# Moving part of an attention prologue from VectorE to GpSimd, the next scores a place later, and constant matmuls in front of the first products

## The reference

```python
q_d, k_d, v_d = mean over groups of 4 positions
out_up = repeat(softmax(scale * q_d @ k_d.T) @ v_d, 4)          # "down" part
scores = where(abs(i - j) < 4, scale * q @ k.T, -1e9)           # "local" part
x = out_up + softmax(scores) @ v                                # 2304 tokens x 512
x = (silu(x @ w_gate) * (x @ w_val)) @ w_out                    # 512 -> 1536 -> 512
h = x @ w_in
out = (maximum(h, 0) + alpha * minimum(h, 0)) @ w_out2          # 512 -> 2048 -> 512
```

## Time and profile before

| | |
|---|---|
| time, median of 3 runs | 984.84 us (984.21 to 985.62) |
| profiled execution | 983.52 us |
| its span, first to last instruction | 981.7 us |
| instructions | 20376 |
| TensorE busy | 952.8 us |
| VectorE busy | 549.7 us |
| ScalarE busy | 247.0 us |
| GpSimd busy | 134.1 us |

### The profile page before, as it was taken

The page is one execution under the profiler, slowest core; times in us unless marked ns, Lnnn a source line. Parts: engine busy times, 40 slices in busy tenths (PEclk is TensorE's granted clock), DMA queues, the critical chain, the costliest instruction groups (busy, mean ns, idle before and its releaser), DMA issues.

```text
span 981.7 us, 20376 instructions
## 1 busy us (share of the span) xinstructions
PE 952.8 (97%) x7912; PEld 889.7 (91%) x7912; DVE 549.7 (56%) x1171; ACT 247.0 (25%) x631; POOL 134.1 (14%) x151
## 2 busy tenths in 40 slices
PE   5899999899998999999999999999999999999998
PEld 3799999799997999999999999999999999999997
DVE  8777666566665666666564554444444444444443
ACT  3444222222221322222223541111111111111111
POOL 5576010010100101000013850000000000000000
PEclk9999999999999999999999999999999999999999
DMA  8465221221211211312105530010010100100000
GB/s 257 138 189 160 81 70 49 66 68 48 85 57 41 92 49 40 102 58 76 48 13 174 163 119 2 1 65 1 0 64 0 43 21 0 64 0 0 32 0 33
DMA packets 31735, 63.07 MB, mean 64 GB/s; under 512 B 2992, under 2 KB 14256, under 8 KB 31664
## 3 DMA queue, kind: packets, MB, share of 16 engines
q1 hardware_dynamic: 31664, 62.02, 20.0%
HBM read 52.57 MB, written 9.44 MB: 63 GB/s over the span
## 4 chain that ended last, share of the span: by engine, by line
PE 90%; DVE 3%; DMA 2%; issue 2%; POOL 2%; ACT 1%; SPq 0%; DVEq 0%; ACTq 0%; POOLq 0%
PE ps L975 50%; PE ps L1012 20%; PE ps L995 14%; PE ps L930 2%; DMA w_raw<-w 2%; PE ps L878 1%; POOL w_lo L428 1%; PE ps L886 1%; PE ps L938 1%; PE ps L916 1%; DMA qk<-qk 0%; DVE h_lo L806 0%; DVE qk_d_early L646 0%; DVE turned_alone L712 0%; DVE turned_one L712 0%
## 5 line engine op out<-in xcount | busy, mean ns | idle before, releaser
L975 PE MATMUL ps<-x_hi,w_hi 128*128 128x288 f32 x768 | 234.3, 305 | 0.7 <-DVE gated L816 0.2
L975 PE MATMUL ps<-x_lo,w_hi 128*128 128x288 f32 x768 | 228.7, 298 | 0.0
L975 PE MATMUL ps<-x_hi,w_lo 128*128 128x288 f32 x768 | 227.6, 296 | 0.0
L552 ACT CAST h_hi<-hidden 128x288 fp32r<-128x288 f32 (+1 forms) x192 | 90.9, 473 | 405.6 <-DVE hidden L843 332.0
L806 DVE TENSOR_TENSOR h_lo<-hidden,h_hi 128x288 fp32r<-128x288 f32 (+1 forms) x192 | 112.2, 585 | 70.0 <-ACT h_hi L552 66.8
L975 PEld LDWEIGHTS ps<-x_hi,w_hi 128*128 128x128 f32 x768 | 146.0, 190 | 4.8 <-issue 1.1
L841 DVE TENSOR_SCALAR gated<-ps,alpha_sb 128x384 f32<-128x384 f32 x96 | 59.3, 617 | 159.5 <-PE ps L975 159.5
L975 PEld LDWEIGHTS ps<-x_hi,w_lo 128*128 128x128 f32 x768 | 146.4, 191 | 0.0
L975 PEld LDWEIGHTS ps<-x_lo,w_hi 128*128 128x128 f32 x768 | 146.4, 191 | 0.0
L995 PE MATMUL ps<-h_hi,w_hi 128*128 128x288 f32 x384 | 115.6, 301 | 0.1
L1012 PE MATMUL ps<-w_lo,h_hi 128*128 128x512 f32 x288 | 113.2, 393 | 0.0
(11 more groups left out here) (123 smaller groups left out, 1423.1 us busy)
## 6 DMA issues: line engine op xcount, KB each, us to landing
w_raw<-w SPq DMA_DIRECT2D x68, 256.0 KB, 2.7
qk<-qk SPq DMA_DIRECT2D x30, 436.0 KB, 3.5
vsrc_one<-vsrc SPq DMA_DIRECT2D x29, 288.0 KB
vwin<-vwin SPq DMA_DIRECT2D x30, 192.0 KB, 2.3
y_t<-y_sb SPq DMA_DIRECT2D x8, 576.0 KB, 3.4
x_raw<-y_t SPq DMA_DIRECT2D x6, 768.0 KB, 5.6
out<-y_sb SPq DMA_DIRECT2D x5, 768.0 KB, 4.1
qk_early<-qk SPq DMA_DIRECT2D x2, 436.0 KB, 6.1
```

The lines of the kernel that those rows point to most:

```text
L552: nc.scalar.copy(h_hi[r][:, 0:width], hidden[r][:, 0:width]).then_inc(h_hi_ready, 1)
L975: mm = nc.tensor.matmul(out_ps, w[:, piece, 128 * k:128 * k + 128], x_parts[low][:, k, :], start=(k == 0 and n == 0), stop=(k == KC - 1 an ...
```

## The change

- **GpSimd averages v** of pairs 2 and 3 of the prologue (`POOL_AVERAGES`), each in two additions: halves of the groups of four in place (512 elements a partition), then the two results (256 elements). They stand ahead of `normalise(2)` and behind `normalise(3)` in its queue.
- **GpSimd makes the low parts of x** of pairs 0, 1 and 2, between the low parts of the weight pieces. TensorE waits for them with a semaphore of their own (`x_lo_early`) ahead of the loop.
- **VectorE's order** in the prologue: `turn_local` of pairs 1, 2 and 3 and the fourth `reciprocals` come forward, `average_v` of pairs 0 and 1 stands behind; `average_qk` for the next block comes behind the last low part of x. `add_up` waits for the one before it.
- **The scores of pair 0 of every next block** come at place 1 instead of 0, behind the first gate products; its maxima, exponentials and reciprocals also go a place later. `average_v`, `turn_local`, `transpose_down` and `pair_outputs` keep their places.
- **Constant matmuls**: 8 ahead of the outputs of pair 3 in the prologue, 12 behind them, into a PSUM bank that is free.

```diff
+WARM_LAST_PAIR, WARM_FIRST_GATE = 8, 12
+POOL_AVERAGES = 2
+def scored_at(k):
+    return 0 if k else 1
...
 GpSimd, prologue:
-            for k in range(PAIRS):
-                normalise(k, k, 0)
-            for j in range(POOL_PIECES, EARLY_PIECES):
-                split_rest(j)
+            def average_v(k):
+                pool.wait_ge(vsrc_in[k], 16)
+                v = vsrc_sb[0][k]
+                nc.gpsimd.tensor_tensor(v[:, :, :, 0:2], v[:, :, :, 0:2], v[:, :, :, 2:4], ALU.add).then_inc(v_halved, 1)
+                pool.wait_ge(v_halved, k - POOL_AVERAGES + 1)
+                nc.gpsimd.tensor_tensor(v_d[0][k][:, :, :], v[:, :, :, 0], v[:, :, :, 1], ALU.add).then_inc(v_averaged_pool, 1)
+            def split_x_lo(k):
+                pool.wait_ge(x_hi_ready, k + 1)
+                nc.gpsimd.tensor_tensor(x_lo[0][:, k, :], x_f32[0][k][:, :], x_hi[0][:, k, :].bitcast(F32), ALU.subtract).then_inc(x_lo_early, 1)
+            normalise(0, 0, 0)
+            normalise(1, 1, 0)
+            average_v(2)
+            normalise(2, 2, 0)
+            normalise(3, 3, 0)
+            average_v(3)
+            split_rest(2)
+            for k in range(PAIRS - 1):
+                split_x_lo(k)
+                split_rest(3 + k)
...
 ScalarE, VectorE, TensorE, attention(a, half, p):
-                if at == 1:
+                if at == scored_at(k) + 1:
...
-                if at == 0:
+                if at == scored_at(k):
...
-                if at == 2:
+                if at == scored_at(k) + 2:
...
 VectorE, add_up:
+                if not mode and k:
+                    dve.wait_ge(x_added, k)
...
 VectorE, prologue:
             reciprocals(0, 2, 0)
-            average_v(0, 0)
             turn_local(0, 1, 0)
             reciprocals(0, 3, 0)
+            average_v(0, 0)
+            turn_local(0, 2, 0)
             average_v(0, 1)
             add_up(0, 0, 0)
-            turn_local(0, 2, 0)
-            average_v(0, 2)
-            split_x_lo(0, 0, 0, 0)
+            turn_local(0, 3, 0)
             add_up(0, 1, 0)
-            turn_local(0, 3, 0)
-            average_v(0, 3)
-            split_x_lo(1, 0, 1, 0)
             add_up(0, 2, 0)
-            average_qk(1, 0)
-            split_x_lo(2, 0, 2, 0)
             add_up(0, 3, 0)
             split_x_lo(3, 0, 3, 0)
+            average_qk(1, 0)
+            dve.sem_inc(v_averaged, PAIRS - POOL_AVERAGES)
+            dve.sem_inc(x_lo_ready, PAIRS - 1)
...
 TensorE, pair_outputs:
-                pe.wait_ge(v_averaged, q + 1)
+                if mode or k < POOL_AVERAGES:
+                    pe.wait_ge(v_averaged, q + 1)
+                else:
+                    pe.wait_ge(v_averaged_pool, k - POOL_AVERAGES + 1)
...
 TensorE, prologue:
+            def keep_busy(times):
+                for _ in range(times):
+                    nc.tensor.matmul(bank(scores_ps[0][0][1])[:, 0:2 * DOWN], ident_bf[:, :], band[:, :, :, :].rearrange("p h t c -> p (h t c)"),
+                                     start=True, stop=True)
...
             pair_outputs(0, 2, 0)
+            keep_busy(WARM_LAST_PAIR)
             pair_outputs(0, 3, 0)
+            keep_busy(WARM_FIRST_GATE)
...
             pe.sem_inc(h_used, 2)
+            pe.wait_ge(x_lo_early, PAIRS - 1)
```

More of the change, by code:

```diff
@@ L220, in build @@
         v_averaged = sem("v_averaged")
+        v_halved = sem("v_halved")
+        v_averaged_pool = sem("v_averaged_pool")
+        x_lo_early = sem("x_lo_early")
         turned_zeroed = sem("turned_zeroed")
```

## The result

| | before | after |
|---|---|---|
| median of 5 runs | 984.5 us (984.21 to 985.62) | 978.84 us (976.87 to 980.64) |
| profiled execution, span | 983.52, 981.7 us | 976.87, 975.1 us |

The page of the changed kernel, busy time, answers to the earlier trace rows: TensorE has 2.9 us less of it, with 20 matmuls more.

A forecast was written before the change was run, and what follows sets the result against it. It took TensorE, busy 97% of the span, to bound the kernel. Terms 0.65 + 0.96 - 1.3 + 1.5 + 0.3 - 2.7 = -0.6 us, applied to the 984.84 median, gave 984.2 us, range 981.2 to 987.0.

The forecast's parts named there:

- the jumps: Loop's two jumps back: products between the idles save 0.6 us each, half the clock falls go; -2.7 us (0 to -4.4).
- The first product: End of the prologue: the big products start at 35.45 (34.9 to 36.0) against 34.80, +0.65 us.
- the eight constants on the path: Prologue, before pair 3's outputs: eight constant matmuls no longer fill a wait and cost 1.3 us (0.7 to 1.9).
- The small operation behind the third reciprocals: VectorE's prologue: a small addition waits for GpSimd's v sums of pair 2, losing 0.4 us (0 to 1.2).
- The output matmuls: End of the prologue on TensorE: pair 2's outputs take 1.34 and then 0.75 us.
- The clock in the first products and block 0: Prologue's end and block 0: fewer slow products, -1.3 us (0 to -2.1); later scores delay TensorE, +1.5 us (0.9 to 2.0).
- The wait ahead of the down transposes: Block 0, pair 0: scores come 12 products later, transposes stay at place 5, so TensorE waits 1.5 us (0.9 to 2.0).
- Blocks 1 to 6: Later blocks, before place 5: later scores cost nothing to 0.1 us each, +0.3 us together.
- Scores at the end: Scores moved behind the first products must still be done, at the fast clock: +0.96 us.
- the clock pays in full: Rival: constant matmuls bring the fast clock before the first product, no slow clock follows a jump; 981.2 us, chance 0.27.
- The second: Rival at the loop's jumps: an instruction block ends just after the jump, so the -2.7 is gone; 986.9 us, chance 0.19.
- The third: Rival in the prologue: GpSimd's sums take 2.8 us or hit VectorE twice, products at 36.3; 985.1 us, chance 0.12.

The follow-up runs named there:

- e1_pad_before: The kernel before plus 34 tiny constant matmuls (68 instructions) in TensorE's first prologue wait: 977.51 us against 985.09, ratio 0.9923.
- e6_block_ends_early: The changed kernel plus 12 tiny matmuls (24 instructions) in TensorE's first wait: 986.08 us, ratio 1.0026 to the kernel before.
- e4_scores_first: The changed kernel with the scores of pair 0 back at place 0 in every block: 986.01 us, ratio 1.0009 to the kernel before.
- e17_best_four: The changed kernel with earlier v averages, scores back at place 0, constants 8 and 6, padding and four raw weight buffers: 970.91 us, ratio 0.9871 to the kernel before.
- e5_scores_later: The kernel before with only the scores, exponentials and reciprocals of pair 0 a place later: 978.94 us against 983.52, ratio 0.9959.
- e3_no_constant: The changed kernel without its 20 constant matmuls: 979.62 us, ratio 0.9942 to the kernel before.

## Why the prediction was wrong

**The step that failed is the jumps: -2.7 us put, -5.22 measured** (outside its bounds of 0 to -4.4). The mechanism held: blocks of instructions, the second one a near-fixed time behind the first, some ten products between. (The Trainium skill, Runtime: NRT & Kernel Launch, section on instruction fetch mechanics, gives 256 instructions a block. By that, 68 more instructions ahead of the loop put its top just past the boundary that stood 67 behind it, and e1_pad_before agrees: the idle of 2.33 among the scores is gone.) Its size was wrong twice. I gave the idle -0.6 a jump, as products for score matmuls one to one in time, with the second block a fixed time behind the first; it was -1.34 and -1.60. At the first jump eleven products and the start and end of the pipeline hold 1.69 us of TensorE's time where 0.73 stood, and the second block came 2.69 us after the first work instead of 3.06 (2.41 and 3.05 at the second jump; 2.4 to 3.3 over all kernels, and no run shows why). And I gave half of the clock falls; both went. At 12 to 14 slow products each, that is some 1.4 us a fall. Idles and falls make -5.7 together. The 0.5 too many are what the pipeline takes: eleven products cost 11 x 0.13 = 1.44 us in a dense row, 0.25 less at each jump than the 1.69 that they stand for between two idles.

**The first product, +0.65 put, -0.23 measured**, both from the third reciprocals on. VectorE's idle of 1.00 (0.9 put) and the eight constants on the path (1.39 from start to start, 1.3 put) came as written. The small operation behind the third reciprocals was stretched as forecast (L722, 0.63, so 0.46 lost against 0.4 put), but by luck: the two sums took 1.04 and 0.64 and were over at 19.03, since their source had landed 1.6 us before the time put for it, and what L722 met was the normalising of GpSimd, which ended at 20.12:

```profile
19.45 0.67 POOL L460 TENSOR_TENSOR down_early<-down_early,first_inv 72x288 f32<-72x288 f32 x1
```

The output matmuls did not come as written: I added 1.34 and 0.75 for a pair, but in a dense row they are 1.64 from start to start (29.77 to 31.41), 0.45 less, twice. That is the whole miss of 0.88. Another 0.98 us of the profiled difference was an earlier start, which no step could have.

**The clock in the first products and block 0, +0.2 put, -1.28 measured.** The clock paid in full: it was up at 32.4, ahead of the first product, so that the old slow stretch, 20 products in the 4.9 us to 39.7, is gone: at 0.13 each they take 2.6, so 2.3 (I had put the whole cost at 2.1 and the saving at 1.3). The wait ahead of the down transposes was 1.04 (1.5 put). A second wait of 1.04 that I had not seen, ahead of L913, makes up for that: there a tanh on ScalarE is late behind a weight cast that waited 2.05 us for its piece, and VectorE's addition, which the scores want, stands behind what the tanh feeds. The old block 0 had 0.9 us of small waits of its own, the new one 0.2 beside the two. That makes -0.9 of the -1.28; the rest is within what block 0 differs by from one execution to another. TensorE's waits between 34.2 and 104 us in the kernel before:

```profile
PE ps L916 <- POOL down_one L450: 0.4, 2, 0.2
PE ps L886 <- DVE x_f L721: 0.3, 1, 0.3
PE ps L975 <- DVE gated L816: 0.2, 1, 0.2
```

**Blocks 1 to 6, +0.3 put:** no wait there, 0. **Scores at the end, +0.96 put:** +1.04.

**The rivals.** The first, the clock pays in full, was the right one for the clock, and its 981.2 still too slow by the second idles. The second is real, but 24 instructions away: the change left 27 in the block, e6_block_ends_early 3. The third didn't happen: the sums took 1.76 us from first to last, and the products stood at 33.59. Where I said "nothing shows where a block begins", the trace did: in the earlier trace rows the second idle comes behind 4 + 28 score matmuls, so the boundary could be counted, and each added instruction moves it by one. What I priced as a side effect was nearly all of the change: 5.2 of the 6.7 us between the two traces, and another 1.0 is the earlier start. e1_pad_before has as much without any of the rest.

## What to carry to other kernels

When a loop's jump back shows two idles of "issue", count the instructions between them: that is what is left of the block at the loop's top, and anything added ahead of the loop on that engine moves it. Try a few dozen small instructions in a wait of the prologue before rearranging work, and judge any rearrangement with the boundary held still, or its gain is that of the boundary. Price a jump with the clock fall that may follow it, and price rows of matmuls from start to start.

## What the runs showed of the hardware

- A jump back costs TensorE 1.3 to 2.3 us of idle time here if the block behind the target is whole, 2.2 to 3.0 in two pieces if eleven products stand between, 3.8 to 4.0 if only score matmuls do, and 5.2 to 5.7 if three instructions do.
- After such a stretch the granted clock can read 0.50 for 3.4 us; it read so for 6.8 at both jumps of e6_block_ends_early and at the first of e4_scores_first. With score matmuls first behind the jump it fell at 13 of 20 traced jumps, once behind an idle of 1.34 us (e17_best_four). With products first it fell at 1 of 18 (e5_scores_later, behind 2.27 us), e6_block_ends_early left out.
- VectorE's subtraction with two operands in SBUF took 0.41 to 0.46 us alone. Where it met GpSimd it ended 0.3 us behind the end of one of GpSimd's operations. Mostly that was the first one that it met: 1.3 us beside an operation of 1.27, also where GpSimd had more of them in a row, of which the next then took 1.5. Ten times it was a later one: 1.6 to 3.3 with four buffers for weight pieces, and 4.28 in e3_no_constant. No run shows what decides.
- GpSimd's sum of 256 elements with a step of 16 bytes took 0.64 us, the one of 512 with halves in place 1.04. The Trainium skill, GPSIMD Engine Reference, section on performance pitfalls, gives half as much again for each element with such a step. This trace shows nothing of that size: a straight line through the normalising of 192 and of 288 elements (0.51 and 0.66 us), an estimate, gives 0.61 for 256 and 1.01 for 512.
